# Rounding and splitting the transposed probabilities over two PSUM banks at once, in a bucketed attention and MLP kernel

## Chip, cores and metric

One core of one Trainium2 chip. The metric is the device time of one execution, in microseconds; the median of three runs of the kernel before is 785.12 us (782.92 to 787.24).

## What is computed

Attention with a hash mask over 2 batches, 8 heads, 768 tokens and head size 64, then two MLP blocks on the result (model size 512). Shortened from the reference:

```python
q_bits = (einsum('bhsd,dk->bhsk', q, proj) > 0)      # 6 bits; k_bits alike
mask = q_bucket[:, :, :, None] == k_bucket[:, :, None, :]
scores = where(mask, scale * q @ k.T, -1e9)
attn = exp(scores - max) / (sum + 1e-9)
x = attn @ v                                         # heads side by side: 768 x 512 per batch
h = maximum(x @ w_in, 0); u, v = halves of h; v = normalise(v)
x = (u * (w_spatial @ v + b_spatial)) @ w_out
out = x + maximum(normalise(x) * g_ln @ w_ch1, 0) @ w_ch2
```

All is in float32. Products are made from operands split in two: a high part rounded to the fast matmul format (fp32r) and a low part, the exact rest. So each matrix that goes into a product is written twice, high by ScalarE or GpSimd, low by VectorE or GpSimd.

## The kernel before

The program is written engine by engine, and the order of each engine's work is fixed in the code; semaphores tie them. A batch is attention (8 heads, as 4 pairs), then a spatial MLP, then a channel MLP of 16 slices. The change lies in the attention.

A **tile** is 128 queries against all 768 keys of a head: 6 tiles a head, 48 a batch, 96 in all. A step `n` of the loop over a pair's 12 tiles does, on each engine in this order:

- TensorE (`steps`, L554): wait for the masked scores of tile n+1, make the scores of tile n+2 (`scores`, L490, lines 498 and 499, four products of 384 columns, two PSUM banks), transpose the 128 x 768 exponentials of tile n (`transposes`, L521, line 528, six transposes of 128 x 128), in steps 4, 5, 10 and 11 hash products for a later head (`hash_planes`, L502, line 508), every third step a turn of a finished output (line 551), and four products with V for an earlier group of three tiles (`times_v`, L532, lines 540 and 542).
- ScalarE (`steps`, L810): the exponential of tile n+1 (line 788), then the high part of tile n's transposed probabilities (`PTh`, through the helper of line 783), and every third step a copy and a scaling of outputs (lines 793 and 801).
- VectorE (`steps`, L968): mask and row minimum of tile n+2 (`masked_scores`, line 935), on some steps the sums for a softmax denominator or the hash buckets (`sum_bits`, line 949), then the low part of tile n (`pt_lo`, L952, line 957), then the mask of tile n+4 (`make_mask`, line 927).

The transposed probabilities of one tile fill two PSUM banks, 4 and 5 (`PT_BANK`), 384 of 512 columns in each, three transposes a bank. There is no second pair of banks for them. They are handed round in halves j = 0 and 1, one bank each: `transposes` waits for `pt_split` of the tile before in that bank, writes three transposes and signals `pt_ready`; ScalarE rounds that bank into `PTh` and signals `pt_hi`; VectorE subtracts and writes `PTl`, and signals `pt_split`.

For most heads the bucket numbers of the keys must be spread over all partitions, as a row. After `sum_bits` (in steps 6 and 12) the sync engine writes them to memory (line 281) and reads them back broadcast (`kb`, line 286); the mask of the next head's first tile waits for this. The last transfer of each kind in a batch follows the bucket sum of tile 36's step; the last head's tiles are 42 to 47. In the last pair of a batch there are no hash products and the last tile's products with V are made apart (`last_times_v`, L591): all high halves, then all low halves. GpSimd splits Q, K, V and the weights meanwhile.

Of the kernel before, what the change touches and what calls it, by code (L numbers as in the profile page):

```python
# [11 lines left out]
P = 128  # L12
# [3 lines left out]
ALU = mybir.AluOpType  # L16
# [4 lines left out]
START = 2  # L21
# [3 lines left out]
def bucket_attention_mlp_kernel(nc, bucket_rows, qkT, qqT, kkT, v, proj, w_in, w_spT, b_sp, w_out, g_ln, w_ch, consts, out):  # L25
# [5 lines left out]
    T = S // P  # L31
    HC = T // 2
    C = HC * P
# [11 lines left out]
    with ctx:  # L45
        def sem(name):
            return ctx.enter_context(nc.semaphore(name))
# [4 lines left out]
        def put(name, shape, dt):  # L52
            width = 2 if dt == BF16 else 4
            for n in shape[1:]:
                width *= n
            t = nc.alloc_sbuf_tensor_at(name, shape, dt, offset=cursor[0])
            cursor[0] += (width + 31) // 32 * 32
            return t
# [6 lines left out]
        ident = cst[:, 0:P]  # L65
# [48 lines left out]
        Pe = [put(f"Pe{s}", [P, S], F32) for s in range(2)]  # L114
        PTh = [put(f"PTh{s}", [P, T, C], F32R) for s in range(2)]
        PTl = [put(f"PTl{s}", [P, T, C], F32R) for s in range(2)]
# [31 lines left out]
        bank = ctx.enter_context(nc.psum_tensor("bank", [P, 8, 512], F32))  # L148
        PT_BANK, O_BANK, MISC, H_BANK = 4, 6, 7, 6
# [36 lines left out]
        pt_ready = sem("pt_ready")  # L186
        pt_hi = sem("pt_hi")
        pt_split = sem("pt_split")
# [40 lines left out]
        def f32(ap):  # L229

            return ap.bitcast(F32)
# [251 lines left out]
        def _(pe):  # L483
# [37 lines left out]
            def transposes(g, n):  # L521

                pe.wait_ge(exp_done, g + 1)
                for j in range(2):
                    pe.wait_ge(pt_split, START + 2 * g + j - 1)
                    for r in range(HC):
                        k = HC * j + r
                        last = nc.tensor.transpose(bank[:, PT_BANK + j, r * P:(r + 1) * P],  # L528
                                                   Pe[n % 2][:, k * P:(k + 1) * P], ident)
                    last.then_inc(pt_ready, 1)  # L530

            def times_v(g0, c, tiles):  # L532

                s, m = (c // 2) % 2, c % 2
                if tiles[0] == 0:
                    if m == 0:
                        pe.wait_ge(head_split, g0 + T * (c // 2 + 1))
                    pe.wait_ge(pt_split, START + 2 * (g0 + HC * (c + 1)))
                for k in tiles:
                    nc.tensor.matmul(bank[:, O_BANK, 0:C], Vs[s][:, k, :], PTh[m][:, k, :],  # L540
                                     start=(k == 0), stop=False)
                    last = nc.tensor.matmul(bank[:, O_BANK, 0:C], Vs[s][:, k, :], PTl[m][:, k, :],  # L542
                                            start=False, stop=(k == T - 1))
                if tiles[-1] == T - 1:
                    last.then_inc(av_done, 1)
# [45 lines left out]
            def last_times_v(b):  # L591

                g = TILES * PAIRS * (b + 1)
                dst = bank[:, LAST_O_BANK, 0:C]
                pe.wait_ge(pt_split, START + 2 * g - 2)
                for j in range(2):
                    pe.wait_ge(pt_hi, 2 * g - 1 + j)
                    for k in range(HC * j, HC * (j + 1)):
                        nc.tensor.matmul(dst, Vs[1][:, k, :], PTh[1][:, k, :], start=(k == 0), stop=False)
                for j in range(2):  # L600
                    pe.wait_ge(pt_split, START + 2 * g - 1 + j)
                    for k in range(HC * j, HC * (j + 1)):
                        last = nc.tensor.matmul(dst, Vs[1][:, k, :], PTl[1][:, k, :], start=False, stop=(k == T - 1))
                last.then_inc(av_done, 1)

            def finish(b):

                cc = 2 * HB * (b + 1)
                pe.wait_ge(o_scaled, START + cc - 2)
                turn(cc - 2)  # L610
                last_times_v(b)
                pe.wait_ge(x_done, START + cc - 1)
                for t in range(HC):
                    x_transposes(b, t)
                pe.wait_ge(o_scaled, START + cc - 1)
                turn(cc - 1)
# [164 lines left out]
        def _(act):  # L781
            def rounded(dst, src, done):
                nc.scalar.activation(dst, src, ACT.Copy).then_inc(done, 1)  # L783

            def exps(g, n):

                act.wait_ge(masked, g + 1)
                nc.scalar.activation(Pe[n % 2][:, :], Sm[n % 2][:, :], ACT.Exp, bias=neg_max[:, n:n + 1],  # L788
                                     scale=-1.0, accum_out=sums[:, n:n + 1]).then_inc(exp_done, 1)

            def copy_o(cc, o_bank=O_BANK):
                act.wait_ge(av_done, AV_START + cc + 1)
                nc.scalar.activation(OTs[:, :], bank[:, o_bank, 0:C], ACT.Copy).then_inc(o_copied, 1)

            def scale_o(cc, c):

                act.wait_ge(x_done, START + cc)
                act.wait_ge(rden_done, cc + 1)
                act.wait_ge(o_turned, cc + 1)
                for t in range(HC):  # L800
                    last = nc.scalar.activation(On[:, t, :], bank[:, MISC, t * P:(t + 1) * P], ACT.Copy,  # L801
                                                scale=rden[:, c % 2, t:t + 1])
                last.then_inc(o_scaled, 1)

            def copy_buckets(b, s):
                act.wait_ge(kb_mm, 2 * b + s + 1)
                nc.scalar.activation(kb[s][:, :].rearrange("q (p t) -> q t p", t=T),
                                     misc16[:, 0:S].rearrange("q (t p) -> q t p", t=T), ACT.Copy).then_inc(kb_copied, 1)

            def steps(b, i, which, last):  # L810
                pair = PAIRS * b + i
                g0, cc0, hh0 = TILES * pair, 4 * pair, 2 * pair
                for n in which:
                    if n + 1 < TILES or not last:
                        exps(g0 + n + 1, (n + 1) % TILES)
                    if last and n == 10:
                        scale_o(cc0 + 1, 1)
                    if n % HC == 0 and n >= 2 * HC:
                        copy_o(cc0 + n // HC - 2)
                    if last and n == 11:  # L820
                        copy_o(cc0 + 2)
                    m, r = (n // HC) % 2, n % HC
                    if r == 0:
                        act.wait_ge(av_done, AV_START + cc0 + n // HC - 1)
                    for j in range(2):
                        act.wait_ge(pt_ready, 2 * (g0 + n) + j + 1)
                        rounded(PTh[m][:, HC * j:HC * (j + 1), r * P:(r + 1) * P],
                                bank[:, PT_BANK + j, 0:C].rearrange("p (k q) -> p k q", k=HC), pt_hi)
                    if n % HC == 0 and n >= 2 * HC and not (last and n == 9):
                        scale_o(cc0 + n // HC - 2, n // HC - 2)  # L830
                    if n == 1:
                        copy_buckets(b, 1)
# [28 lines left out]
            with act.Fori(0, B) as b:  # L861
                copy_buckets(b, 0)
                act.wait_ge(g_in, 16)
                exps(TILES * PAIRS * b, 0)
                steps(b, 0, range(4), False)
                with act.Fori(0, PAIRS - 1) as i:
                    steps(b, i, range(4, TILES + 4), False)
                steps(b, PAIRS - 1, range(4, TILES), True)
                scale_o(2 * HB * (b + 1) - 2, 2)

# [12 lines left out]
                for j in range(2 * KU):  # L883
# [3 lines left out]
                    d, c = j // 2, j % 2  # L887
                    act.wait_ge(u_mm, 2 * KU * b + j + 1)
                    nc.scalar.activation(UT[:, d, c * C:(c + 1) * C], bank[:, j % HC, 0:C], ACT.Relu).then_inc(u_relu, 1)
                for j in range(2 * KU):  # L890
                    c, d = j // KU, j % KU
# [22 lines left out]
        def _(dve):  # L914
# [36 lines left out]

            def pt_lo(g, n):  # L952
                m, r = (n // HC) % 2, n % HC
                for j in range(2):
                    dve.wait_ge(pt_hi, 2 * g + j + 1)
                    part = (slice(None), slice(HC * j, HC * (j + 1)), slice(r * P, (r + 1) * P))
                    nc.vector.tensor_tensor(PTl[m][part], bank[:, PT_BANK + j, 0:C].rearrange("p (k q) -> p k q", k=HC),  # L957
                                            f32(PTh[m][part]), ALU.subtract).then_inc(pt_split, 1)

            def denominator(cc0, c):  # L960
                nc.vector.tensor_scalar(den[:, c % 2, :], sums[:, HC * c:HC * (c + 1)], 1e-9, None,
# [242 lines left out]
```

## Time and profile before

| | |
|---|---|
| median of 3 runs | 785.12 us (782.92 to 787.24) |
| span of the profiled execution, first to last instruction | 774.0 us |
| own time of that execution | not listed apart; the runs shown lie 8.9 to 13.2 us above its span |
| TensorE matmul / weight load busy | 725.7 / 658.3 us |
| VectorE, ScalarE, GpSimd busy | 386.2, 319.2, 292.8 us |
| instructions | 12055 |
| mean granted TensorE clock | 0.965 |

The profile follows one execution. A group of rows names the line, engine, operation and tiles, how often it ran, its time and what ended the idle time before it. Busy shares are averages over stages: attention of batch 0 lies at about 14 to 172 us of the span, that of batch 1 at about 397 to 553.

### The profile page before, as it was taken

How to read it: one execution, taken by the hardware profiler on the slowest of the kernel's cores; microseconds unless marked ns; L12 is line 12 of the kernel's file. 1: busy time of each engine (PE TensorE's matmuls, PEld its weight loads, DVE VectorE, ACT ScalarE, POOL GpSimd, SP SyncE). 2: the span in 40 equal slices, each digit the busy share in tenths (PEclk: the TensorE clock that was granted, in tenths of full speed). 3: DMA queues.
4: the chain of work that ended last, by engine and by line, in shares of the span. 5: the costliest groups of instructions: out<-in, count | busy, mean ns of one | idle time of the engine just before them, and what ended most of it. 6: DMA issues, size and time to landing. Idle time of an engine off the chain costs nothing.

```text
span 774.0 us, 12055 instructions
## 1 busy us (share of the span) xinstructions
PE 725.7 (94%) x3864; PEld 658.3 (85%) x3864; DVE 386.2 (50%) x860; ACT 319.2 (41%) x688; POOL 292.8 (38%) x295
## 2 busy tenths in 40 slices
PE   5888898999899999999989899889999999999998
PEld 4778787887898898998978888779889988999987
DVE  4778878874834511111157787668643453111112
ACT  4667766683412311111147676668732132111110
POOL 5353535607720144434643344441210003454351
PEclk9999999899999999999988899988999999999999
DMA  5143434202300021121432333333000000212212
GB/s 202 62 110 82 109 81 102 46 17 75 117 28 1 0 74 63 54 81 54 149 106 61 81 83 81 81 81 95 1 28 1 1 0 28 81 54 59 76 54 82
DMA packets 21122, 51.15 MB, mean 66 GB/s; under 512 B 4192, under 2 KB 7904, under 8 KB 21088
## 3 DMA queue, kind: packets, MB, share of 16 engines
q1 hardware_dynamic: 19744, 45.22, 20.7%
q0 software_dynamic: 1344, 5.51, 2.1%
q8 instruction: 17, 0.28, 0.1%
q14 instruction: 17, 0.14, 0.1%
HBM read 47.56 MB, written 3.16 MB: 66 GB/s over the span
## 4 chain that ended last, share of the span: by engine, by line
PE 74%; DMA 10%; DVE 7%; issue 6%; ACT 2%; DVEq 1%; SPq 0%; ACTq 0%
PE bank L697 12%; PE bank L723 11%; PE bank L486 6%; PE bank L488 6%; PE bank L487 6%; PE bank L702 6%; PE bank L528 6%; DMA kb<-bucket_rows 6%; PE bank L727 5%; DMA bucket_rows<-kb_col 4%; PE bank L508 4%; PE bank L498 2%; PE bank L499 2%; PE bank L540 2%; PE bank L542 2%
## 5 line engine op out<-in xcount | busy, mean ns | idle before, releaser
L1065 DVE SCALAR_TENSOR_TENSOR Hl<-bank,Hh 128x384 fp32r<-128x384 f32 x64 | 35.6, 557 | 208.7 <-ACT Hh L856 208.6
L528 PE MATMUL bank<-cst,Pe 128*128 128x128 f32 x576 | 95.6, 303 | 30.0 <-DVE PTl L957 29.5
L856 ACT ACTIVATE Hh<-bank 128x384 fp32r<-128x384 f32 x64 | 31.5, 492 | 216.1 <-PE bank L702 216.1
L528 PEld LDWEIGHTS bank<-cst,Pe 128*128 128x128 f32 x576 | 72.8, 154 | 51.0 <-DVE PTl L957 39.0
L347 POOL TENSOR_SCALAR W1h<-w_raw 128x512 fp32r<-128x512 f32 x32 | 19.8, 618 | 246.2 <-PE bank L702 206.4
L788 ACT ACTIVATE Pe<-Sm,neg_max 128x768 f32<-128x768 f32 x96 | 90.5, 942 | 42.4 <-DVE neg_max L935 40.3
L935 DVE CUSTOM_DVE_ANT_0 Sm<-bank,mask 128x768 f32<-128x768 f32 x96 | 91.2, 950 | 33.0 <-PE bank L499 29.4
L783 ACT ACTIVATE PTh<-bank 128x384 fp32r<-128x384 f32 x192 | 87.1, 493 | 45.2 <-PE bank L528 41.9
L957 DVE TENSOR_TENSOR PTl<-bank,PTh 128x384 fp32r<-128x384 f32 x192 | 97.5, 546 | 7.6 <-ACT PTh L783 7.2
L697 PE MATMUL bank<-XNh,W1l 128*128 128x384 f32 x256 | 86.9, 340 | 0.0
L697 PE MATMUL bank<-XNh,W1h 128*128 128x384 f32 x256 | 86.7, 339 | 0.0
L498 PE MATMUL bank<-KH,Qs 128*128 128x384 f32 x192 | 72.0, 375 | 6.5 <-DVE neg_max L935 3.3
L927 DVE TENSOR_SCALAR mask<-kb,qb 128x768 bf16<-128x768 bf16 x96 | 59.4, 620 | 31.0 <-DMA kb<-bucket_rows 25.8
L540 PE MATMUL bank<-PTh,Vs 128*128 128x384 f32 x180 | 71.3, 396 | 0.0
L499 PE MATMUL bank<-KL,Qs 128*128 128x384 f32 x192 | 70.9, 369 | 0.0
L723 PE MATMUL bank<-W2l,Hh 128*128 128x512 f32 x180 | 70.9, 394 | 0.0
L723 PE MATMUL bank<-W2h,Hh 128*128 128x512 f32 x180 | 70.8, 393 | 0.0
L542 PE MATMUL bank<-PTl,Vs 128*128 128x384 f32 x180 | 63.6, 353 | 0.0
L356 POOL TENSOR_TENSOR X<-On 128x192 f32<-128x192 f32 (+1 forms) x32 | 20.3, 634 | 96.6 <-ACT On L801 96.6
L702 PE MATMUL bank<-XNl,W1h 128*128 128x384 f32 x256 | 54.7, 334 | 0.0
L727 PE MATMUL bank<-W2h,Hl 128*128 128x512 f32 x180 | 51.2, 392 | 0.0
L697 PEld LDWEIGHTS bank<-XNh,W1h 128*128 128x128 f32 x256 | 48.1, 188 | 3.5 <-ACT XNh L850 0.7
(118 smaller groups left out, 1476.7 us busy)
## 6 DMA issues: line engine op xcount, KB each, us to landing
w_raw<-w_ch SPq DMA_DIRECT2D x32, 512.0 KB, 3.5
qk_raw<-qkT SPq DMA_DIRECT2D x16, 384.0 KB, 4.9
q_raw<-qqT SPq DMA_DIRECT2D x16, 384.0 KB, 5.3
k_raw<-kkT SPq DMA_DIRECT2D x16, 384.0 KB, 6.3
v_raw<-v SPq DMA_DIRECT2D x16, 192.0 KB, 5.1
out<-X SPq DMA_DIRECT2D x12, 256.0 KB, 2.1
kb<-bucket_rows SPq DMA_DIRECT2D x12, 192.0 KB, 4.8
w_raw<-w_spT POOLq DMA_DIRECT2D x6, 384.0 KB, 3.4
```

What stands on the lines that cost most here:

```text
L498: nc.tensor.matmul(dst, q, KH[s][:, c * C:(c + 1) * C], start=True, stop=False)
L499: last = nc.tensor.matmul(dst, q, KL[s][:, c * C:(c + 1) * C], start=False, stop=True)
L528: last = nc.tensor.transpose(bank[:, PT_BANK + j, r * P:(r + 1) * P], Pe[n % 2][:, k * P:(k + 1) * P], ident)
L540: nc.tensor.matmul(bank[:, O_BANK, 0:C], Vs[s][:, k, :], PTh[m][:, k, :], start=(k == 0), stop=False)
L697: nc.tensor.matmul(bank[:, h_bank, 0:C], w1[s][:, k * P:(k + 1) * P], XNh[:, k, c * C:(c + 1) * C], start=(k == j == 0), stop=False)
L702: last = nc.tensor.matmul(bank[:, h_bank, 0:C], W1h[s][:, k * P:(k + 1) * P], XNl[:, k, c * C:(c + 1) * C], start=False, stop=(k == KD - 1))
L723: nc.tensor.matmul(bank[:, t, :], Hh[s][:, t * P:(t + 1) * P], w2[s][:, :], start=first and k == 0, stop=False)
L727: last = nc.tensor.matmul(bank[:, t, :], Hl[s][:, t * P:(t + 1) * P], W2h[s][:, :], start=False, stop=False)
L783: nc.scalar.activation(dst, src, ACT.Copy).then_inc(done, 1)
L788: nc.scalar.activation(Pe[n % 2][:, :], Sm[n % 2][:, :], ACT.Exp, bias=neg_max[:, n:n + 1], scale=-1.0, accum_out=sums[:, n:n + 1]).then_i ...
L935: nc.vector.tensor_tensor_reduce(halves(Sm[n % 2][:, :]), bank[:, 2 * (n % 2):2 * (n % 2) + 2, 0:C], halves(mask[n % 3][:, :]), -SCALE, 3. ...
L957: nc.vector.tensor_tensor(PTl[m][part], bank[:, PT_BANK + j, 0:C].rearrange("p (k q) -> p k q", k=HC), f32(PTh[m][part]), ALU.subtract).th ...
```

## The change

Rounding (ScalarE) and splitting (VectorE) of a tile's transposed probabilities become one operation each, over both banks, where there were two each, one for a bank. TensorE waits once for the split of the tile before, writes six transposes and signals once; each of the three semaphores counts one per tile. The last product of a batch waits for its high and low parts whole.

```diff
             def transposes(g, n):
 
                 pe.wait_ge(exp_done, g + 1)
-                for j in range(2):
-                    pe.wait_ge(pt_split, START + 2 * g + j - 1)
-                    for r in range(HC):
-                        k = HC * j + r
-                        last = nc.tensor.transpose(bank[:, PT_BANK + j, r * P:(r + 1) * P],
-                                                   Pe[n % 2][:, k * P:(k + 1) * P], ident)
-                    last.then_inc(pt_ready, 1)
+                pe.wait_ge(pt_split, START + g)
+                for k in range(T):
+                    last = nc.tensor.transpose(bank[:, PT_BANK + k // HC, k % HC * P:(k % HC + 1) * P],
+                                               Pe[n % 2][:, k * P:(k + 1) * P], ident)
+                last.then_inc(pt_ready, 1)
...
-                    pe.wait_ge(pt_split, START + 2 * (g0 + HC * (c + 1)))
+                    pe.wait_ge(pt_split, START + g0 + HC * (c + 1))
...
-                pe.wait_ge(pt_split, START + 2 * g - 2)
+                pe.wait_ge(pt_split, START + g - 1)
+                pe.wait_ge(pt_hi, g)
                 for j in range(2):
-                    pe.wait_ge(pt_hi, 2 * g - 1 + j)
...
+                pe.wait_ge(pt_split, START + g)
                 for j in range(2):
-                    pe.wait_ge(pt_split, START + 2 * g - 1 + j)
...
-                    for j in range(2):
-                        act.wait_ge(pt_ready, 2 * (g0 + n) + j + 1)
-                        rounded(PTh[m][:, HC * j:HC * (j + 1), r * P:(r + 1) * P],
-                                bank[:, PT_BANK + j, 0:C].rearrange("p (k q) -> p k q", k=HC), pt_hi)
+                    act.wait_ge(pt_ready, g0 + n + 1)
+                    rounded(PTh[m][:, :, r * P:(r + 1) * P].rearrange("p (j k) q -> p j k q", j=2),
+                            bank[:, PT_BANK:PT_BANK + 2, 0:C].rearrange("p j (k q) -> p j k q", k=HC), pt_hi)
...
             def pt_lo(g, n):
                 m, r = (n // HC) % 2, n % HC
-                for j in range(2):
-                    dve.wait_ge(pt_hi, 2 * g + j + 1)
-                    part = (slice(None), slice(HC * j, HC * (j + 1)), slice(r * P, (r + 1) * P))
-                    nc.vector.tensor_tensor(PTl[m][part], bank[:, PT_BANK + j, 0:C].rearrange("p (k q) -> p k q", k=HC),
-                                            f32(PTh[m][part]), ALU.subtract).then_inc(pt_split, 1)
+                dve.wait_ge(pt_hi, g + 1)
+                part = (slice(None), slice(None), slice(r * P, (r + 1) * P))
+                nc.vector.tensor_tensor(PTl[m][part].rearrange("p (j k) q -> p j k q", j=2),
+                                        bank[:, PT_BANK:PT_BANK + 2, 0:C].rearrange("p j (k q) -> p j k q", k=HC),
+                                        f32(PTh[m][part]).rearrange("p (j k) q -> p j k q", j=2),
+                                        ALU.subtract).then_inc(pt_split, 1)
```

## Rows read from the trace of the kernel before

**Rows 1.** The page: TensorE's busy time, its granted clock by slice; the mean clock.

```profile
PE 725.7 (94%) x3864; PEld 658.3 (85%) x3864; DVE 386.2 (50%) x860; ACT 319.2 (41%) x688; POOL 292.8 (38%) x295
...
PEclk9999999899999999999988899988999999999999
...
core 0: 774.0 us, clock 0.965
```

**Rows 2.** Windows: length, busy us (instructions) by engine, clock, DMA share, GB/s.

```profile
152.00:168.00 16.00, 15.98 (x107) 14.43 (x105) 15.28 (x38) 15.30 (x40) 2.43 (x4) 1.00 0.12 42
96.40:99.80 3.40, 3.40 (x15) 3.31 (x15) 1.41 (x3) 0.68 (x3) 3.24 (x3) 0.53 0.00 0
```

**Rows 3.** Timeline, VectorE, fast steps: start, us, engine, line, operation, tiles.

```profile
161.40 0.96 DVE L935 CUSTOM_DVE_ANT_0 Sm<-bank,mask 128x768 f32<-128x768 f32 x1
...
162.28 1.02 DVE L957 TENSOR_TENSOR PTl<-bank,PTh 128x384 fp32r<-128x384 f32 x2
...
163.54 0.95 DVE L935 CUSTOM_DVE_ANT_0 Sm<-bank,mask 128x768 f32<-128x768 f32 x1
```

**Rows 4.** Timeline, one handover from split to transposes to rounding.

```profile
128.39 1.01 DVE L957 TENSOR_TENSOR PTl<-bank,PTh 128x384 fp32r<-128x384 f32 x2
...
128.99 0.31 PEld L528 LDWEIGHTS bank<-cst,Pe 128*128 128x128 f32 x3 [0.45 <-DVE PTl L957]
...
129.73 0.86 ACT L783 ACTIVATE PTh<-bank 128x384 fp32r<-128x384 f32 x2
```

**Rows 5.** Timeline, TensorE in a step with hash products.

```profile
113.89 1.01 PE L528 MATMUL bank<-cst,Pe 128*128 128x128 f32 x6 [1.61 <-DVE PTl L957]
114.73 1.40 PE L508 MATMUL bank<-planes,qk_raw 128*128 128x12 f32 x6
...
117.48 0.82 PE L528 MATMUL bank<-cst,Pe 128*128 128x128 f32 x6
```

**Rows 6.** Waits: VectorE on the bucket row; us in total, times, longest.

```profile
DVE mask L927 <- DMA kb<-bucket_rows: 25.8, 11, 3.6
```

**Rows 7.** Timeline: six unbroken transposes; a rounding and the split that waited for it.

```profile
161.06 0.82 PE L528 MATMUL bank<-cst,Pe 128*128 128x128 f32 x6
...
28.15 0.86 ACT L783 ACTIVATE PTh<-bank 128x384 fp32r<-128x384 f32 x2
28.65 1.02 DVE L957 TENSOR_TENSOR PTl<-bank,PTh 128x384 fp32r<-128x384 f32 x2 [1.88 <-ACT PTh L783]
```

**Rows 8.** Groups by shape: rounding and low part, 384 and 512 columns.

```profile
L783 ACT ACTIVATE PTh<-bank 128x384 fp32r<-128x384 f32 x192 | 87.1, 493 | 45.2 <-PE bank L528 41.9
...
L783 ACT ACTIVATE XTh<-bank 128x512 fp32r<-128x512 f32 x12 | 6.9, 601 | 3.5 <-PE bank L588 3.5
...
L957 DVE TENSOR_TENSOR PTl<-bank,PTh 128x384 fp32r<-128x384 f32 x192 | 97.5, 546 | 7.6 <-ACT PTh L783 7.2
...
L1029 DVE TENSOR_TENSOR XTl<-bank,XTh 128x512 fp32r<-128x512 f32 x12 | 7.9, 673 | 4.8 <-ACT XTh L783 4.8
```

**Rows 9.** Timeline: last bucket sum and last splits of each batch, and a rounding.

```profile
143.51 0.88 ACT L783 ACTIVATE PTh<-bank 128x384 fp32r<-128x384 f32 x2 [0.53 <-PE bank L528]
...
144.31 0.18 DVE L949 TENSOR_REDUCE kb_col<-weighted 128x6 bf16<-128x36 f32 x1
...
170.66 1.02 DVE L957 TENSOR_TENSOR PTl<-bank,PTh 128x384 fp32r<-128x384 f32 x2 [0.47 <-ACT PTh L783]
...
526.78 0.18 DVE L949 TENSOR_REDUCE kb_col<-weighted 128x6 bf16<-128x36 f32 x1
...
552.07 1.02 DVE L957 TENSOR_TENSOR PTl<-bank,PTh 128x384 fp32r<-128x384 f32 x2 [0.48 <-ACT PTh L783]
```

**Rows 10.** Timeline: bucket sum, the mask that waits for its row, the next transposes.

```profile
83.35 0.18 DVE L949 TENSOR_REDUCE kb_col<-weighted 128x6 bf16<-128x36 f32 x1
...
92.33 0.42 DVE L927 TENSOR_SCALAR mask<-kb,qb 128x768 bf16<-128x768 bf16 x1 [1.59 <-DMA kb<-bucket_rows]
...
94.17 1.01 PE L528 MATMUL bank<-cst,Pe 128*128 128x128 f32 x6 [1.01 <-DVE PTl L957]
```

## Prediction

> **What bounds the kernel now.** I read the page first. TensorE is busy for 94% of the span and its granted clock is near full [rows 1], so it seems to be the bound everywhere. That is an average over stages. The change touches the attention stage alone, so I looked there. In a stretch of it without any transfer or hashing, TensorE, VectorE and ScalarE are each busy for over 15 of 16 us [rows 2]: three engines are about level. The order of events shows who ends last. VectorE starts a masked score tile every 163.54 - 161.40 = 2.14 us, with the two splits of L957 (1.02 us) directly behind it [rows 3]. Those fast steps are bound by VectorE's own work, about 2.15 to 2.4 us each.
>
> Under them lies a loop over the two banks of transposed probabilities: the transposes of tile n+1 into a bank wait for the split of tile n out of it. Because there are two banks and each half hands over alone, three engines work on one tile at once. After the first split starts at 128.39 the transposes of the next tile start at 128.99, while the second split still runs, and their first half is being rounded at 129.73, before all six are through [rows 4]. Each bank's own loop: 0.55 split, 0.05 to the transposes (128.39 + 0.55 = 128.94 against 128.99), 0.74 to the rounding, 0.49 rounding, 0.04 to the split; 1.87 us. It fits under 2.14 with 0.27 to spare.
>
> Two other kinds of step exist. Where the hash products run, TensorE's own work sets the step: 117.48 - 113.89 = 3.59 us, with 1.40 us of hash products after the transposes [rows 5]. And once per head VectorE waits (before a mask) for the bucket row to come back from memory: 25.8 us over 11 waits, 2.35 us each [rows 6].
>
> **The new loop, step by step.** The change leaves all work in place. It takes away one rounding, one split and one signal of each kind per tile (96 tiles), and makes both banks one unit.
>
> Transposes to rounding. Today 0.74 us with three transposes. Six unbroken ones take 0.82 us, the last of them 0.27 us long, so (0.82 - 0.27)/5 = 0.11 apart [rows 7]; three more add 0.33. New: 1.07 us.
>
> Rounding. 384 columns take 493 ns, 512 take 601 [rows 8], 0.84 ns a column; 768 columns: 493 + 384 x 0.84 = 0.81 us. No row shows this engine reading over two banks. Lower bound: a pair's 0.88 us from start to end [rows 9] less one fixed part, 0.49 - 384 x 0.00084 = 0.17, so 0.71. Upper bound: two of today's, 0.99.
>
> Rounding to split: 28.15 + 0.49 = 28.64, split at 28.65 [rows 7]; elsewhere some 0.04. I take 0.04.
>
> Split. 384 columns take 546 ns, 512 take 673, so about 1.0 ns a column; 768 make 0.945 us. VectorE already reads a pair of banks in one operation of 768 columns, in 0.96 us [rows 3], so two banks in one pattern cost nothing special there. Bounds: 1.02 less a fixed part of 0.546 - 0.384 = 0.16, so 0.86, and two of today's, 1.09.
>
> Split to transposes: 0.05.
>
> Sum: 0.05 + 1.07 + 0.81 + 0.04 + 0.945 = 2.92 us per tile, with the bounds 2.73 and 3.25. It is one closed loop, since there is only one pair of banks: transposes wait for the whole split before, rounding for all six, split for the whole rounding. VectorE's mask and masked scores, ScalarE's exponential and TensorE's products and scores lie beside it: a step without hashing is 2.14 us of VectorE's time and about as much of TensorE's. So a fast step becomes 2.92 instead of some 2.2: **+0.7 us**, and all three engines idle in it.
>
> What the change gives back is small. A pair of splits runs from start to end in 1.02 us, the second beginning before the first has ended; one of 768 columns would take 0.945. That is 0.07 us of VectorE's time per tile, worth at most 96 x 0.07 = 7 us if VectorE still set every step. Where the loop sets it, it is worth nothing more than is already in the 2.92.
>
> The Trainium skill has rules for both sides. "VectorE: DVE Perf Modes", section on the TRN2 errata, gives a fixed 120 cycles at 0.96 GHz to each operation out of PSUM, to be paid once by a large tile; by an estimate from it the merged split would save 125 ns, not 70, and the kernel would gain 12 us at most. "Perfetto Trace Analysis", section Optimizing Scalar/DVE Operations, says that operations which hold up other engines are better broken up. That one speaks against the change, and the order of events in this trace agrees with it, since transposes already run under the second split.
>
> **Where the longer loop shows.**
>
> (a) The end of each batch's attention. From the last bucket sum that feeds a transfer there is no hash product any more and hardly a wait. In batch 0 the stretch runs from 144.31 to the last split's end, 170.66 + 1.02 = 171.68: 27.37 us; in batch 1 from 526.78 to 552.07 + 1.02 = 553.09: 26.31 us [rows 9]. It holds twelve splits. The first now ends at 143.51 + 0.33 + 0.81 + 0.04 + 0.945 = 145.63, 1.32 us after the start (143.51 is where its rounding begins today), and eleven loops follow: 1.32 + 11 x 2.92 = 33.44 us. That is +6.1 in batch 0 and +7.1 in batch 1: **+13.2**.
>
> (b) The steps behind the transfer. After a head's bucket sum (83.35) the row needs until 92.33, 8.98 us, whatever the engines do [rows 10]. Three fast steps lie in it. They grow by 3 x 0.77 = 2.3 us, and the wait they eat into is 2.35 us on average. So they are **hidden**; the cover is the transfer's latency, and if it were gone they would cost 12 x 2.3 = 28 us.
>
> (c) The hash steps, 3.59 us, are longer than the loop, which stays hidden under them. But the first of them begins with the transposes that wait for a split: today these start after the first half of it (94.17 [rows 10]), and then after the whole, 0.945 - 0.546 = 0.40 later; unbroken, they take 0.82 instead of 1.01 [rows 5, 7], so 0.19 comes back. **+0.2** per head over ten heads: +2.
>
> (d) The opening of each batch: two steps before the first hash products where the later start (0.40) counts twice, less 0.2: +0.6 in each, **+1.2**.
>
> After the attention nothing changes, but the last product now starts its high half after the whole rounding; 0.3 us later than by halves at most, already inside the error of (a).
>
> Sum: 13.2 + 2 + 1.2 = 16.4 us on the profile's span of 774.0. The runs shown have a median of 785.12, so 11.1 us lie around the span, and I carry that over: 785.1 + 16.4 = **801.5 us**.
>
> **The clock** is left at what it was. It matters, however: for 3.4 us after such a wait the profile has the granted clock at 0.53, that is mostly at 1.2 GHz, and TensorE busy for all 3.40 [rows 2]; before the fall it had stood idle and then run hash products. The mean over the span is 0.965 [rows 1], so 2 x 0.035 x 774 = 54 us at half clock, and what is lost there is at most 27 us. The change alters TensorE's gaps in both senses: shorter ones at the transfer, new ones of about 0.6 us in each fast step.
>
> **The rivals.**
>
> Clock falls more often, or the transfer does not cover. The new gaps lead to some 8 more stretches of 3.4 us at half clock (each up to 1.7 us lost), or half of the 28 us of (b) comes out. Against it: even at 2.92 us a fast step keeps TensorE at some 75% of its time. Then 801.5 + 14 = 815 us. Chance 0.15.
>
> Clock falls less often, because the wait at the transfer is mostly filled. A third of the 27 us comes back: 801.5 - 9 = 792 us. Chance 0.08.
>
> Faster. VectorE is the bound of the fast steps and gets shorter by 0.07 us per tile. It decides only if the loop, 2.92, falls under 2.14, for which rounding and transposes would have to overlap across tiles; with one pair of banks they can't. It would give 785.1 - 7 = 778 us. Chance 0.04. (The Trainium skill's first rule above is this rival; by its figure the time would be 773.)
>
> The loop is hidden everywhere, or the merged operations do not come out as one piece of work longer than the old pair (the change does not do what it says), so that gain and loss cancel: 785 us. Chance 0.04.
>
> The forecast has 0.69.
>
> **How the numbers follow.** The loop's bounds, 2.73 and 3.25, give (a) 22 x -0.19 = -4 and 22 x 0.33 = +7; with (c) and (d), each 1 us either way, the forecast's own range is 796 to 810. Taking in the clock cases it is 791 to 818. About 0.5% (4 us) is what a measurement of this kernel can tell. Faster 0.04, the same 0.05 (the hidden case and the low edge of the lesser-clock case), slower 0.91.
>
> **What would show it.** In the changed profile: one rounding of about 0.81 us and one split of about 0.95 us per tile, 96 of each; in the stretch 152 to 168 starts of the masked scores 2.9 us apart instead of 2.14, with VectorE waiting for the rounding and TensorE for the split; the idle time before the mask of each new head down from 25.8 us to near nothing at an unchanged 9 us from bucket sum to mask; hash steps still 3.6 us. It is wrong if the fast steps stay under 2.4 us, if the rounding over two banks takes over 1.1 us, or if the mean granted clock moves by more than 0.01.

## The result and the profile after

The changed kernel takes **804.11 us** (median of four runs, 803.73 to 806.9) beside 786.18 us for the kernel before (782.92 to 788.76): ratio 1.0233, 95% interval 1.0184 to 1.0282. Run again beside the kernel before, on two chips, it came to 795.57 beside 781.78 us (ratio 1.0184, 1.0108 to 1.0259) and 798.74 beside 781.33 us (1.0233, 1.0157 to 1.031). So it is slower by about 2%, 14 to 18 us. With the executions left out that lie over 1.5% above the fastest of their kernel, these two differences are 18 and 13 us, so the size is known to a few us only.

The page of the changed kernel, the rows that answer to [rows 1] and [rows 8]:

```profile
PE 729.5 (91%) x3864; PEld 663.0 (83%) x3864; DVE 383.5 (48%) x764; ACT 307.2 (38%) x592; POOL 294.8 (37%) x295
...
PEclk9999987999999999999988799899999999999999
...
L526 PE MATMUL bank<-cst,Pe 128*128 128x128 f32 x576 | 92.0, 302 | 52.4 <-DVE PTl L953 52.4
...
L781 ACT ACTIVATE PTh<-bank 128x768 fp32r<-128x768 f32 x96 | 78.0, 812 | 106.3 <-PE bank L526 106.3
L953 DVE TENSOR_TENSOR PTl<-bank,PTh 128x768 fp32r<-128x768 f32 x96 | 91.8, 956 | 51.1 <-ACT PTh L781 50.9
```

And of the kernel before, the transposes:

```profile
L528 PE MATMUL bank<-cst,Pe 128*128 128x128 f32 x576 | 95.6, 303 | 30.0 <-DVE PTl L957 29.5
```

VectorE and ScalarE do less: 2.7 and 12.0 us less busy, 96 instructions fewer each. A wide rounding takes 812 ns, a wide split 956 ns; 810 and 945 were forecast. What grew is waiting: VectorE stood 7.2 us before a split for its rounding and now stands 50.9; TensorE stood 29.5 us before the transposes for a split and now 52.4 (its idle time in all, span less busy time, went from 48.3 to 72.4 us); ScalarE 41.9 us for transposes and now 106.3. All three wait, each for the one before it in the loop. In the steps without hash products no engine is the bound: the loop is.

The same fast steps as in [rows 3], of the changed kernel, from the timeline:

```profile
162.57 0.95 DVE L932 CUSTOM_DVE_ANT_0 Sm<-bank,mask 128x768 f32<-128x768 f32 x1
...
163.36 0.81 ACT L781 ACTIVATE PTh<-bank 128x768 fp32r<-128x768 f32 x1 [0.34 <-PE bank L526]
...
164.20 0.96 DVE L953 TENSOR_TENSOR PTl<-bank,PTh 128x768 fp32r<-128x768 f32 x1 [0.67 <-ACT PTh L781]
...
165.31 0.85 PE L526 MATMUL bank<-cst,Pe 128*128 128x128 f32 x6 [0.59 <-DVE PTl L953]
165.40 0.95 DVE L932 CUSTOM_DVE_ANT_0 Sm<-bank,mask 128x768 f32<-128x768 f32 x1
...
166.19 0.81 ACT L781 ACTIVATE PTh<-bank 128x768 fp32r<-128x768 f32 x1 [1.11 <-PE bank L526]
```

The loop can be read off in one round: rounding 163.36 to 164.17, split 164.20 to 165.16, transposes from 165.31, rounding again at 166.19. That is 2.83 us, the distance of the masked scores too (165.40 - 162.57). Nothing of one tile lies beside anything of the next within the loop. In the window 155 to 171 us TensorE is busy for 12.55 of 16 us at a granted clock of 1.00, where the kernel before has 15.77.

The end stretches, as in [rows 9], of the changed kernel:

```profile
151.83 0.18 DVE L946 TENSOR_REDUCE kb_col<-weighted 128x6 bf16<-128x36 f32 x1
...
184.23 0.96 DVE L953 TENSOR_TENSOR PTl<-bank,PTh 128x768 fp32r<-128x768 f32 x1 [1.58 <-ACT PTh L781]
...
548.18 0.19 DVE L946 TENSOR_REDUCE kb_col<-weighted 128x6 bf16<-128x36 f32 x1
...
579.91 0.96 DVE L953 TENSOR_TENSOR PTl<-bank,PTh 128x768 fp32r<-128x768 f32 x1 [1.59 <-ACT PTh L781]
```

33.36 us (151.83 to 185.19) and 32.69 us (548.18 to 580.87), where there were 27.37 and 26.31: **+12.4 us** together. Of the 22 distances between their splits 21 are 2.77 to 2.91 us; the other, 3.40 us, holds a mask of 1.66 us.

The resume after the transfer, as in [rows 10]:

```profile
83.09 0.18 DVE L946 TENSOR_REDUCE kb_col<-weighted 128x6 bf16<-128x36 f32 x1
...
87.18 1.77 DVE L924 TENSOR_SCALAR mask<-kb,qb 128x768 bf16<-128x768 bf16 x1
...
93.32 0.42 DVE L924 TENSOR_SCALAR mask<-kb,qb 128x768 bf16<-128x768 bf16 x1 [2.47 <-DMA kb<-bucket_rows]
...
95.64 0.84 PE L526 MATMUL bank<-cst,Pe 128*128 128x128 f32 x6 [2.22 <-DVE PTl L953]
```

From the mask to the transposes it takes 2.32 us, before 94.17 - 92.33 = 1.84: the late start of step (c), 0.48 where 0.40 was forecast. But the row itself came later too: 93.32 - 83.09 = 10.23 us after the bucket sum, where it had been 8.98. Over the ten heads that wait for a row in either kernel it is 8.92 us on average before, and 9.69, 9.66 and 9.05 us in three executions of the changed kernel.

Where the two profiled executions are compared as a whole (774.0 and 801.9 us) the difference is 27.9 us, 10 more than the medians'. Wherever both were recorded, an execution's time is some 1.8 us over its span. So the profiled execution of the kernel before was a quick one, about 776 us, while that of the changed kernel, 803.73 us, was an ordinary one. The 27.9 us are 12.4 in the end stretches, 12.6 in ten heads and 2.9 in the openings. The end stretches repeat to 0.1 us from execution to execution of the changed kernel (33.35 and 32.69, 33.37 and 32.68 us in two more). What varies are the heads in between, the arrival of the row, and the clock. The last six bucket sums of a batch stand 20.51 and 20.64 us apart on average in the kernel before; in three executions of the changed kernel 21.81 and 21.86, 21.70 and 21.80, 20.64 and 21.21. The third of these has a span of 792.0 us: 18.0 over the kernel before, with 12.4 in the end stretches, 3.5 in ten heads and 1.8 in the openings, at a mean clock of 0.970 against 0.965.

### The profile page after: what moved, and what is told of

Same layout as the page of the kernel before. It is cut to its first block, busy times and chain, and to the rows that moved or that the text cites. A ratio compares the mean times of both kernels' runs of the same rounds, so it can differ in the third digit from the quotient of the medians.

```text
span 801.9 us, 11447 instructions
## 1 busy us (share of the span) xinstructions
PE 729.5 (91%) x3864; PEld 663.0 (83%) x3864; DVE 383.5 (48%) x764; ACT 307.2 (38%) x592; POOL 294.8 (37%) x295
## 4 chain that ended last, share of the span: by engine, by line
PE 72%; DVE 10%; DMA 9%; ACT 5%; issue 3%; SPq 0%; DVEq 0%; ACTq 0%
PE bank L695 11%; PE bank L721 10%; PE bank L526 7%; PE bank L486 6%; PE bank L488 6%; PE bank L487 6%; PE bank L700 6%; PE bank L725 5%; DVE PTl L953 5%; DMA kb<-bucket_rows 4%; PE bank L508 4%; DMA bucket_rows<-kb_col 4%; ACT PTh L781 3%; PE bank L498 2%; PE bank L538 2%
## 5 line engine op out<-in xcount | busy, mean ns | idle before, releaser
L526 PE MATMUL bank<-cst,Pe 128*128 128x128 f32 x576 | 92.0, 302 | 52.4 <-DVE PTl L953 52.4
L781 ACT ACTIVATE PTh<-bank 128x768 fp32r<-128x768 f32 x96 | 78.0, 812 | 106.3 <-PE bank L526 106.3
L953 DVE TENSOR_TENSOR PTl<-bank,PTh 128x768 fp32r<-128x768 f32 x96 | 91.8, 956 | 51.1 <-ACT PTh L781 50.9
L924 DVE TENSOR_SCALAR mask<-kb,qb 128x768 bf16<-128x768 bf16 x96 | 61.4, 641 | 28.0 <-DMA kb<-bucket_rows 22.5
L538 PE MATMUL bank<-PTh,Vs 128*128 128x384 f32 x180 | 73.3, 407 | 0.0
L356 POOL TENSOR_TENSOR X<-On 128x192 f32<-128x192 f32 (+1 forms) x32 | 22.8, 713 | 122.4 <-ACT On L799 122.4
```

The source lines that it names most:

```text
L526: last = nc.tensor.transpose(bank[:, PT_BANK + k // HC, k % HC * P:(k % HC + 1) * P], Pe[n % 2][:, k * P:(k + 1) * P], ident)
L953: nc.vector.tensor_tensor(PTl[m][part].rearrange("p (j k) q -> p j k q", j=2), bank[:, PT_BANK:PT_BANK + 2, 0:C].rearrange("p j (k q) -> p ...
```

## The experiments

In all kernels below, the end stretch runs from a batch's last bucket sum of this kind to the end of its last split; head distance is the mean over the five distances between a batch's last six bucket sums, for each batch. Times are medians; the last three columns are of one profiled execution each.

| kernel | time, beside before | ratio (95%) | end stretches | head distance | mean clock |
|---|---|---|---|---|---|
| before (profiled) | 786.18 | | 27.37, 26.31 | 20.51, 20.64 | 0.965 |
| change | 804.11, 786.18 | 1.0233 (1.0184 to 1.0282) | 33.36, 32.69 | 21.81, 21.86 | 0.957 |
| whole handover, two operations | 797.47, 777.69 | 1.0262 (1.022 to 1.0305) | 35.42, 34.29 | 20.31, 20.04 | 0.976 |
| rounding merged only | 783.70, 777.69 | 1.008 (1.0045 to 1.0114) | 30.97, 29.06 | 21.20, 20.51 | 0.965 |
| split merged only | 794.26, 777.69 | 1.0218 (1.0153 to 1.0284) | 31.43, 29.75 | 21.25, 22.21 | 0.953 |
| late transposes only | 795.14, 781.33 | 1.0187 (1.0122 to 1.0252) | 28.74, 27.61 | 22.32, 21.57 | 0.946 |
| before, no row transfer | 741.96, 777.69 | 0.953 (0.9492 to 0.9568) | 27.27, 26.16 | 17.46, 16.80 | 0.984 |
| change, no row transfer | 772.12, 781.78 | 0.9894 (0.9824 to 0.9964) | 33.76, 32.80 | 18.91, 18.32 | 0.989 |
| before, early bucket sum | 759.53, 781.78 | 0.9745 (0.9675 to 0.9815) | 28.30, 26.54 | 18.94, 19.08 | 0.982 |
| change, early bucket sum | 774.63, 781.78 | 0.9919 (0.9882 to 0.9957) | 34.85, 34.01 | 19.15, 18.70 | 0.993 |

In the last two the bucket sum comes a mask and a score tile earlier, so their end stretches begin earlier by that much.

### Is it the wide operation or the handover?

The changed kernel with two roundings and two splits again, one wait and one signal for each pair:

```diff
-                    rounded(PTh[m][:, :, r * P:(r + 1) * P].rearrange("p (j k) q -> p j k q", j=2),
...
+                    for j in range(2):
+                        last_r = nc.scalar.activation(PTh[m][:, HC * j:HC * (j + 1), r * P:(r + 1) * P],
+                                bank[:, PT_BANK + j, 0:C].rearrange("p (k q) -> p k q", k=HC), ACT.Copy)
+                    last_r.then_inc(pt_hi, 1)
...
+                for j in range(2):
...
+                last_s.then_inc(pt_split, 1)
```

> Two roundings and two splits per tile as before, but handed over whole, with one wait and one signal each. Own theory (what costs is the early handover that is lost): the loop is 0.05 + 1.04 + 0.87 + 0.04 + 1.01 = 3.0 us a tile, so fast steps start about 3.0 us apart, the end stretches of the two batches take about 1.3 + 11 x 3.0 = 34.3 us, and the time is about 4 us above that of the change, 808 us. Rival (what costs is something in the wide operations themselves, two banks in one pattern): fast steps stay near 2.2 us and the time near 786 us.

Measured: 797.47 us, ratio 1.0262, end stretches 35.42 and 34.29 us, splits mostly 2.96 us apart in them. The rival is out: without any wide operation the loss is there in full, and at a higher mean clock, 0.972 over four runs beside 0.964 of the kernel before on that chip. It is the handover. The end stretches are 3.7 us above the change's, what merging gives back where the loop decides. It was run again beside the change:

> Whole handover with two operations each, beside the change on one chip: 3 to 5 us above it if only the fixed parts of the operations differ. Rival: level with it or below, with a higher mean clock (0.972 against 0.960), because a busier VectorE shifts TensorE's gaps.

> The change beside its relative with two operations each, on one chip: the time should be 3 to 5 us below that one (end stretches 66.1 against 69.7 us) if the wide operations give back what their rows say and the clock treats both alike. Rival: no difference, or the change is the slower one, because its clock is granted lower.

Measured on one chip: 798.06 us (ratio 1.0188, 1.0121 to 1.0255) and 798.74 us for the change (1.0233, 1.0157 to 1.031). By these medians no difference can be told. But each of the two has one execution far above its others (804.94 and 810.35 us); the medians of the other three are 797.82 and 794.28 us, the 3.5 us that were expected. So it stays open. The mean clock is the higher one in the kernel with two operations, 0.971 against 0.962, as its rival says. The end stretches of the former were 34.48 and 34.18, of the change 33.37 and 32.68 us; 2.6 us in its favour are real in the records, and are lost again in the heads between (21.24 and 21.04 us apart against 20.64 and 21.21 in this pair of executions, 20.31 and 20.04 against 21.81 and 21.86 in the first). The spread of single runs, 792.62 to 810.35 us, is larger than what was looked for, and the heads' difference rests on one execution each.

### One merge at a time

```diff
-                    for j in range(2):
-                        act.wait_ge(pt_ready, 2 * (g0 + n) + j + 1)
-                        rounded(PTh[m][:, HC * j:HC * (j + 1), r * P:(r + 1) * P],
...
+                    act.wait_ge(pt_ready, 2 * (g0 + n) + 2)
+                    rounded(PTh[m][:, :, r * P:(r + 1) * P].rearrange("p (j k) q -> p j k q", j=2),
```

> Only the rounding is one operation over two banks; transposes and splits are handed over by halves as before. Own theory: the loop closes through the second bank, split 1.01 + 0.05 to the last three transposes, 0.7 to the rounding, 0.81 rounding, 0.04: 2.63 us a tile; fast steps 2.6 us apart, end stretches 1.3 + 11 x 2.63 = 30.2 us, about half of the loss: 794 to 797 us. Rival (either merge alone still fits under VectorE's 2.15 us): 784 us or a little below.

Measured: 783.70 us, ratio 1.008 (1.0045 to 1.0114); end stretches 30.97 and 29.06 us, +6.4 together. It is slower, but by 6 us, a third of the change's loss and less than expected (the times expected stood beside a kernel before of 786 us, so 8 to 11 us were meant). Its loop is seen in the end stretches: splits 2.49 to 2.58 us apart in the second batch, where 2.63 was expected, and VectorE waits for roundings, 23.5 us in 52 places in all. All of the loss is in these stretches. The transposes still start after half a split, and the heads between are as before within their spread.

```diff
-                for j in range(2):
-                    pe.wait_ge(pt_split, START + 2 * g + j - 1)
...
+                for j in range(2):
+                    pe.wait_ge(pt_split, START + g)
...
-                    dve.wait_ge(pt_hi, 2 * g + j + 1)
...
+                dve.wait_ge(pt_hi, 2 * g + 2)
```

(and the wide split of the change)

> Only the split is one operation over two banks; roundings are handed over by halves. Own theory: the loop is 0.96 split + 0.05 + 0.74 to the first rounding, about 0.9 for the two roundings, 0.04: 2.65 to 2.7 us; fast steps 2.7 us apart, 794 to 798 us. Rival (the fixed part saved on VectorE counts, since VectorE sets the fast steps): fast steps 2.08 us apart and 778 to 784 us.

Measured: 794.26 us, ratio 1.0218, 17 us over the kernel before where 8 to 12 were expected; end stretches 31.43 and 29.75 us, +7.5 together, splits mostly 2.57 us apart. Almost the same loop as with the merged rounding, yet 10 us more in all. The difference lies in the heads between (21.25 and 22.21 us apart) and in the mean clock, 0.953 against 0.965. In this kernel TensorE's transposes wait for the whole split; in the other they don't. The next experiment takes that alone.

### The late start of the transposes alone

```diff
+                pe.wait_ge(pt_split, START + 2 * g)
                 for j in range(2):
-                    pe.wait_ge(pt_split, START + 2 * g + j - 1)
```

> The kernel before with one edit: all six transposes of a tile wait for both splits of the tile before. Roundings and splits stay two each and are handed over by halves. Own theory: the loop is 1.01 + 0.05 + 0.74 + 0.49 + 0.04 = 2.33 us, hardly over VectorE's own 2.15 to 2.4, so the end stretches grow by under 1 us each; the rest is TensorE's later start into the hash steps, 0.4 us a head, and what the clock makes of it: 3 to 8 us above the kernel before, and the mean clock not above 0.965. Rival (the inner heads of the changed kernel lose by their longer loop alone, a later start of the transposes is harmless): within 2 us of the kernel before.

Measured: 795.14 us, ratio 1.0187 (1.0122 to 1.0252), 14 us over the kernel before where 3 to 8 were expected. The end stretches grow by 1.4 and 1.3 us, not by under 1. The rest is in the heads: 22.32 and 21.57 us apart, 1.4 us a head more than in the profile of the kernel before, where the start itself is only 0.4 later. Its timeline at a resume, TensorE and VectorE, and the windows on either side:

```profile
95.93 0.42 DVE L927 TENSOR_SCALAR mask<-kb,qb 128x768 bf16<-128x768 bf16 x1 [2.32 <-DMA kb<-bucket_rows]
...
98.23 1.06 PE L528 MATMUL bank<-cst,Pe 128*128 128x128 f32 x6 [2.05 <-DVE PTl L957]
...
103.45 0.96 DVE L935 CUSTOM_DVE_ANT_0 Sm<-bank,mask 128x768 f32<-128x768 f32 x1 [2.65 <-PE bank L499]
```

```profile
90.00:98.50 8.50, 5.06 (x33) 4.41 (x34) 6.18 (x14) 4.96 (x12) 3.73 (x5) 1.00 0.79 234
98.70:108.90 10.20, 10.20 (x42) 10.01 (x41) 5.06 (x14) 4.29 (x9) 5.53 (x5) 0.50 0.01 2
```

In the second window TensorE is busy for all of 10.2 us at a granted clock of 0.50 (1.2 GHz). It had been busy for 5.06 of the 8.5 us before. VectorE then waits 2.65 us for scores. Such a long stretch is nothing new, though: the kernel before has two of them beside those of 3.4 us [rows 2]. One is this window of the kernel before:

```profile
516.50:526.50 10.00, 10.00 (x40) 9.81 (x41) 5.33 (x14) 4.12 (x10) 5.37 (x5) 0.50 0.00 0
```

What differs is how many there are. Read in windows of 0.5 us, the profile of the kernel before has ten stretches at half clock, two of them of 10 us, 53 us in all; that of this kernel has thirteen, five of 10 us, 82 us in all. It is no matter of one execution: the four runs had mean clocks of 0.940 to 0.956, against 0.952 to 0.969 over eleven runs of the kernel before on that chip. Reckoned as in the prediction, half of the time at half clock, that is 42 us lost on average against 30: at most 12 of the 14 us. That the edit lowers the mean clock of this kernel is shown; what decides whether a stretch lasts 3.4 or 10.2 us is not, nor why the other kernels with the same late start do not all have the lower clock (0.972 in the whole handover with two operations).

### What the transfer hides

Both kernels without the two transfers of the bucket row. These kernels leave out the spreading of the keys' bucket numbers for all heads but the first two of a batch, whose row their masks use.

```diff
-                sp.dma_start(bucket_rows[bass.ds(hh, 1), :].rearrange("a (p t) -> p (a t)", p=P),
-                             kb_col[:, s, :]).then_inc(row_out, 16)
...
-                sp.wait_ge(row_out, 16 * rows)
-                sp.dma_start(kb[s][:, :], bucket_rows[bass.ds(hh, 1), :].to_broadcast([P, S])).then_inc(row_in, 16)
...
-                    else:
-                        dve.wait_ge(row_in, 16 * (hh - 2 * b - 1))
```

> The kernel before without the two transfers of the bucket row and the waits for them; masks of later heads use the first row that stands in the tile. Own theory: the 2.35 us of waiting per head goes and the steps stand open, about 26 us off: 758 to 764 us. Rival (the hash products and the clock bound the heads anyway): 775 us or more.

> The changed kernel without the two transfers of the bucket row and the waits for them, as in the kernel before without them. Own theory (the transfer hides part of the longer loop): with the cover gone the loop of 2.83 us stands open in four steps of each head, so the two kernels lie 1.5 to 2 us per head further apart than with the transfer: 793 us, 32 us above the kernel before without it. Rival (the transfer hides nothing, the rest of the loss is the clock): the distance stays at 18 us, 780 us.

Measured: 741.96 us, well under the 758 to 764 expected, and 772.12 us. The two kernels lie **30.2 us** apart, near the 32 of the second expectation (though the time is 21 us under its 793) and not the 18 of its rival. They ran on two chips; by their ratios, 0.953 and 0.9894, the distance is 28 us. With the transfer it is 14 to 18, so the transfer does hide some 10 to 16 us of the longer loop. The distance splits as the records say: end stretches 13.1 us, ten head distances of about 1.5 us (17.46 to 18.91, 16.80 to 18.32), 15 us, the openings the rest. The clock has little part in it, 0.984 and 0.989. The kernel before gains 36 us by the missing transfer, 10 more than its waits of 25.8 us [rows 6]: part of it can be the clock, which is 0.984 where it was 0.965. Of the changed kernel, two masks of one head, in time, and what GpSimd does beside the second:

```profile
103.33 0.41 DVE L918 TENSOR_SCALAR mask<-kb,qb 128x768 bf16<-128x768 bf16 x1
...
111.53 1.83 POOL L346 TENSOR_TENSOR Qs<-q_raw,Qs 64x768 fp32r<-64x768 f32 x1
111.76 1.82 DVE L918 TENSOR_SCALAR mask<-kb,qb 128x768 bf16<-128x768 bf16 x1
```

Some masks take over 1.8 instead of 0.41 us. In such a step VectorE alone needs some 3.5 us, more than the loop, and the loop costs nothing: in the changed kernel's own profile the splits on either side of the mask of 1.77 us at 87.18 are 3.52 us apart, and VectorE waits for nothing between them.

### A version that beats both

The kernel before, with the bucket sums right behind the weighing of the bits, one step earlier:

```diff
-                    if n in (T, TILES) and not last:
-                        sum_bits(hh0 + n // T + 1, (n // T + 1) % 2)
...
                     if n in (5, 11) and not last:
                         weigh_bits(hh0 + n // T + 2)
+                        sum_bits(hh0 + n // T + 2, (n // T + 2) % 2)
```

> The kernel before with the bucket sums one step earlier (steps 5 and 11, right behind the weighing of the bits), so that the transfers start earlier by a mask and a masked score tile. Own theory: the transfers start 1.3 to 2.4 us earlier, the waits of 2.35 us mostly go: 765 to 773 us. Rival: the wait only turns into one for hash products or the clock falls, 780 us or more.

> The kernel before with the bucket sums a step earlier, again, for its interval. Own theory: 2 to 3% below the kernel before (760 us), with mean clock 0.97 to 0.98, because the wait for the row falls from 25.8 to some 14 us and TensorE stands less. Rival: a chance of that chip, within 1%.

> The changed kernel with the bucket sums one step earlier. Own theory: the transfer no longer ends last before the next head's masks, the loop of 2.83 us does; a gain smaller than that of the same edit on the kernel before: 788 to 795 us. Rival (the loop never competes with the transfer): the same gain as on the kernel before, 783 us or less.

> The change once more, beside the kernel before on one chip, to see spans and granted clocks of both over several executions. Own theory: 804 us again, 18 us above the kernel before, and the kernel before's own mean clock over several executions is below the 0.965 of its profiled one, since its span of 774.0 was some 10 us under what its median would leave. Rival (the clock takes no part): both clocks equal and constant.

Measured: 759.53 us, ratio 0.9745 (0.9675 to 0.9815), and again 758.15 us, ratio 0.9713 (0.967 to 0.9757): 22 and 23 us, 2.5 to 3% faster than the kernel before and under the 765 to 773 us first expected, and 36 to 41 us faster than the change beside it (795.57 and 798.74 us). The waits of the first of them:

```profile
DVE mask L927 <- DMA kb<-bucket_rows: 13.9, 8, 2.7
```

The wait falls by 12 us, from 25.8 [rows 6]; the time by 22. The mean clock rises to 0.982. With the same edit the change takes 774.63 us, 21 less than without it, where 788 to 795 was expected: the gain is as large as on the kernel before, so the rival of that expectation is nearer. There the wait for the row fell from 22.5 to 6.4 us, and the clock rose to 0.993. The change by itself, run beside it, was 14 us over the kernel before, not 18, and its mean clock over four runs was 0.964 beside 0.962: there it loses its time at no lower clock.

## Why the prediction was right, and where its terms were not

**The loop** was forecast at 2.92 us and is 2.83: 0.81 and 0.96 us for the two wide operations, and 1.03 us from the end of a split to the next rounding, 0.09 less than the sum of 0.05 and 1.07. The other loops came out as they were added up too, each a little shorter: 2.51 for 2.63 (rounding merged), 2.57 for 2.65 to 2.7 (split merged), 2.96 for 3.0 (whole handover, two operations). The bound by neither engine is seen in the waits above. The rounding's width, a fixed part and a slope from two shapes of the same operation, held within 0.01 us, over two banks too. The split's 0.945 was not on its own line: 546 ns at 384 columns and 673 at 512 give 927 ns for 768, 0.03 us under the 956 measured.

**(a)**, +13.2 us, was +12.4 in all three profiled executions of the change, against the one of the kernel before. This is the bulk of the loss. It is the one large term, and it is shown: the splits stand 2.83 us apart there, each waiting for its rounding, with or without wide operations.

**(b)** was right that the transfer covers part of the loop, and wrong in its sizes. The wait was to go to near nothing at an unchanged 9 us from bucket sum to mask; it fell only from 25.8 us to 22.5 (23.1 and 17.1 in two more executions), and the 9 us did change. From a bucket sum to the start of the wait VectorE took 6.37 us on average before and 7.45, 7.35 and 7.33 us in the three executions: 1.0 us more, not 2.3. Between the bucket sum and the mask that needs the row there are two closed loops, not three: the split behind the bucket sum hardly moves, and the third loop ends behind the mask. In some heads a long mask covers one of the two. And the row, taken to need 8.98 us whatever the engines do, came 0.1 to 0.8 us later per head, up to 8 us over ten heads. Why it came later was not tried; the median time of the first transfer to landing was 3.6 us before and 4.2, 3.6 and 3.9 us in the three, that of the second 4.8 us and 4.8, 5.3 and 4.7. Without the cover the cost is not 28 us more but 10 to 16: the change costs 1.5 us per head more, not 2.3.

**(c) and (d)**, 3.2 us together, are what is left of 14 to 18 us after the 12.4: 2 to 6. Their sum was about right, their reasoning was not enough, and that the sum fits is in part luck, since the later row and the openings (1.8 to 3.8 us in the three executions, where (d) had 1.2) are in it. The late start was priced at 0.2 us per head as if only its delay mattered. Taken alone it is worth 14 us, and up to 12 of these can be lost at 1.2 GHz. In the changed kernel it did not cost so much: beside the kernel before on two chips its mean clock was 0.964 against 0.962 on the one, and 0.9615 in both kernels on the other. The terms do not add: late start (14 us) and merged rounding (6) are more than the change that holds both, and the merged split, which holds the late start too, has 17. Why the late start costs so much less in the change stays open.

**The clock** was left as it was, and for the change that was right within what can be told: lower in the profiled executions (0.965 to 0.957), level in the two comparisons just given. The rival in which it falls more often had a chance of 0.15 and would have been the better description of the two partial kernels with late transposes (0.947 against 0.962, and 0.955 against 0.964, means of the runs).

**The base.** The 11.1 us taken to lie around the span were wrong: it is 1.8 us, and the profiled execution was a quick one. Since the sum was added to the median, this did no harm.

**The faster rival**, by which VectorE's shorter work should count, is excluded by the row of it: VectorE's busy time did fall, by 2.7 us, and its waiting rose by more. Of the two rules of the Trainium skill cited ahead, the outcome went the way of that of "Perfetto Trace Analysis", section Optimizing Scalar/DVE Operations; with the whole handover and operations that are not merged the loss is as large. The fixed part of an operation that the other rule counts was seen in the end stretches: a pair of splits takes 1.02 us from start to end and the merged one 0.96, so 0.06 us and not the 125 ns of the estimate.

## What to carry to other kernels

Before two operations on a double buffer are merged, add up the closed loop through that buffer, writer, first reader, second reader and back, once by halves and once whole, and compare both with the busiest engine's time per step; here 1.87 us fitted under 2.14 and 2.83 did not. A merge that saves less than 0.1 us on an engine is worth nothing where it turns three engines that overlap into three that take turns. And look at what the longest wait of a step is tied to: moving a small sum one step ahead of its transfer gave more than any of this took.

## What the runs showed beyond it

- Delaying the start of TensorE's transposes until the whole split is done, with nothing else changed, cost 14 us, up to 12 of them by more time at the lower clock: mean 0.947 against 0.962. A wait on TensorE that looks covered can be paid for there; with wide or whole handovers it was not each time.
- Taking the wait for the row away gave 36 us where the records showed 25.8 us of waiting, and halving it gave 22 for 12. The mean clock rose each time (0.984 and 0.982 from 0.965), which can account for part of the rest. Ratios to one chip's own runs are needed: the kernel before took 777.7 to 786.2 us in its four groups of runs.
- The mask operation, of one shape, takes from 0.4 to over 1.8 us. The profile of the kernel before tells beside what: of the 92 masks that its timeline lists singly all 37 of over 0.5 us lie at the same time as a GpSimd operation, and of the 55 shorter ones 45 have none beside them. No run takes the GpSimd work away to test it.
